# The last 64 keys' high and low parts in one product with V, from block 44 on

## The reference

```
scores = (q @ k.T) / 8
thresh = max(scores, -1) - tau
scores = where(scores >= thresh, scores, -1e9)
attn   = exp(scores - max) ; attn = attn / (sum(attn) + 1e-9)
x      = attn @ v                      -> tokens [2304, 512]
h = x @ w1_in ; x = (h * clip(h + 3, 0, 6) / 6) @ w1_out
h = x @ w2_in ; x = (h * sigmoid(1.702 h))     @ w2_out
```

## Time and profile before

| | us |
|---|---|
| median of the 3 timed runs (1092.23 to 1095.72) | 1092.24 |
| the profiled execution | 1094.09 |
| its span, first to last instruction | 1092.3 |
| PE busy | 1049.8 (96%) |
| DVE busy | 803.6 (74%) |
| ACT busy | 601.6 (55%) |
| POOL busy | 473.4 (43%) |

### The profile page before, as it was taken

One profiled execution on the slowest core, in us unless ns is written; L12 is line 12 of the kernel. 1 busy time (PEld: TensorE's weight loads), 2 busy tenths in 40 slices (PEclk: granted clock), 3 DMA queues, 4 the chain that ended last, 5 costly groups with the idle time before them and its releaser, 6 DMA issues.

```text
span 1092.3 us, 18054 instructions
## 1 busy us (share of the span) xinstructions
PE 1049.8 (96%) x6504; PEld 986.7 (90%) x6504; DVE 803.6 (74%) x1436; ACT 601.6 (55%) x1073; POOL 473.4 (43%) x558
## 2 busy tenths in 40 slices
PE   4888899999999999999999999999999999999998
PEld 3767699999999999899999999998998989898897
DVE  4888978788888878776785747898574798666561
ACT  4888886867777776654451615554251546334240
POOL 3566755455645565435370504146150516324050
PEclk9999999999999999999999999999999999999999
DMA  4446553436335452553225032342303033331302
GB/s 117 126 133 172 146 131 108 111 98 151 91 120 124 133 137 77 128 152 112 83 68 159 16 116 78 101 129 64 110 1 114 22 126 111 101 116 38 108 1 87
DMA packets 102824, 112.41 MB, mean 103 GB/s; under 512 B 28096, under 2 KB 81488, under 8 KB 102736
## 3 DMA queue, kind: packets, MB, share of 16 engines
q1 hardware_dynamic: 102432, 110.97, 35.6%
q10 hardware_dynamic: 304, 0.30, 0.1%
HBM read 78.12 MB, written 33.10 MB: 102 GB/s over the span
## 4 chain that ended last, share of the span: by engine, by line
PE 86%; DVE 6%; issue 3%; ACT 3%; DMA 1%; POOL 1%; SPq 0%; ACTq 0%; DVEq 0%; POOLq 0%
PE score L855 12%; PE score L815 11%; PE mm L815 9%; PE score L736 8%; PE mm L774 7%; PE tr L751 6%; PE tr L855 6%; PE mm L781 6%; PE mm L765 6%; PE score L853 5%; PE tr L815 4%; PE tr L853 2%; PE mm L853 2%; DVE prob L958 2%; PE score L781 2%
## 5 line engine op out<-in xcount | busy, mean ns | idle before, releaser
L1594 POOL TENSOR_TENSOR gd_lo<-act_ring,gd_hi 128x384 fp32r<-128x384 f32 x144 | 157.5, 1114 | 350.1 <-ACT gd_hi L1379 348.3
L1269 ACT ACTIVATE pt_hi<-tr 128x640 fp32r<-128x640 f32 x144 | 101.5, 705 | 99.7 <-PE tr L751 99.2
L950 DVE TENSOR_REDUCE neg_max<-score 128x1 f32<-128x576 f32 x144 | 108.3, 752 | 27.6 <-PE score L736 24.4
L976 DVE TENSOR_TENSOR pt_lo<-tr,pt_hi 128x640 fp32r<-128x640 f32 x144 | 118.2, 821 | 11.2 <-ACT pt_hi L1269 10.4
L736 PE MATMUL score<-k_hi,q_sp 128*128 128x288 f32 x320 | 98.2, 323 | 28.4 <-DVE prob L958 19.5
L1558 POOL TENSOR_SCALAR thresh<-neg_max,tau_abs 128x1 f32<-128x1 f32 x144 | 41.6, 289 | 180.4 <-DVE neg_max L950 179.8
L958 DVE SCALAR_TENSOR_TENSOR prob<-score,thresh,prob 128x576 f32<-128x576 f32 x144 | 116.3, 808 | 0.0
L751 PE MATMUL tr<-ident,prob 128*128 128x128 f32 x720 | 105.8, 279 | 8.5 <-issue 6.8
L1264 ACT ACTIVATE prob<-score,neg_max 128x576 f32<-128x576 f32 x144 | 106.3, 738 | 7.8 <-DVE neg_max L950 7.5
L751 PEld LDWEIGHTS tr<-ident,prob 128*128 128x128 f32 x720 | 83.7, 143 | 19.4 <-issue 18.6
L736 PEld LDWEIGHTS score<-k_hi,q_sp 128*128 128x128 f32 x320 | 62.6, 196 | 39.6 <-DVE prob L958 29.7
(11 more groups left out here) (193 smaller groups left out, 3135.6 us busy)
## 6 DMA issues: line engine op xcount, KB each, us to landing
pair_raw<-x_t_scratch SPq DMA_DIRECT2D x36, 384.0 KB, 3.8
q_raw<-in_qT SPq DMA_DIRECT2D x64, 144.0 KB, 2.8
k_raw<-in_kT SPq DMA_DIRECT2D x62, 144.0 KB, 2.9
raw_a<-in_w_out SPq DMA_DIRECT2D x48, 128.0 KB, 2.2
o_parts_scratch<-o_t SPq DMA_DIRECT2D x32, 160.0 KB, 1.8
x_t_scratch<-x_raw SPq DMA_DIRECT2D x8, 576.0 KB, 3.2
part_t_scratch<-y_out SPq DMA_DIRECT2D x8, 576.0 KB, 3.3
y_ring<-part_t_scratch SPq DMA_DIRECT2D x24, 192.0 KB, 2.7
```

What stands on the lines that cost most here:

```text
L950: dve.tensor_reduce(neg_max[:, r:r + 1], score[:, g % 2, :, 0:HALF], AX.XY, ALU.max, negate=True).then_inc(max_done, 1)
L976: dve.tensor_tensor(pt_place(pt_lo, x), turned_place(x), pt_place(pt_hi, x), ALU.subtract).then_inc(pt_lo_done, 1)
L1269: act.activation(pt_place(pt_hi, x), turned_place(x), ACT.Copy).then_inc(pt_hi_done, 1)
L1594: pool.tensor_tensor(gd_lo[:, u, c, :], act_ring[:, g % 3, :], gd_hi[:, u, c, :], ALU.subtract).then_inc(g_lo_done, 1)
```

## The change

From block 44 on (`stacks`), the tail's two parts share one chunk. POOL copies the last 64 columns of a block's `prob` into the 64 columns behind them (`copy_tail`, new, in POOL's step x + 1 right behind the threshold), so the fifth transpose puts the same 64 keys on partitions 0 to 63 and 64 to 127. PE's turn of such a block waits for that copy. ACT's high part is as before. DVE's low part becomes two instructions: on partitions 64 to 127 of the fifth chunk it writes turned minus high back into `pt_hi`, and on the other four chunks it writes `pt_lo` as before (512 elements per partition, not 640). The fifth chunk of `pt_hi` then holds high parts on top and low parts below; it is multiplied once, in the low part of the group's product: nine matmuls, not ten. V's tail has to stand on both halves too, so `load_v` loads it twice (one DMA more for each head) and the memset of `v_raw` goes.

```
+        def stacks(x):
+            return x >= BATCH_SLOTS + LAG
...
-                sp.dma_start(v_raw[0:TAIL, FULL, :], v[h, full:S, :]).then_inc(v_loaded, 16)
+                for half in range(2):
+                    sp.dma_start(v_raw[half * TAIL:half * TAIL + TAIL, FULL, :], v[h, full:S, :]).then_inc(v_loaded, 16)
...
+                if stacks(x):
+                    pe.wait_ge(tail_copied, x - BATCH_SLOTS - LAG + 1)
...
-                for c in range(CHUNKS):
-                    p_part = (pt_hi, pt_lo)[low]
+                stacked = stacks(group_last(n))
+                for c in range(FULL if stacked and not low else CHUNKS):
+                    p_part = pt_lo if low and not (stacked and c == FULL) else pt_hi
...
-            dve.memset(v_raw[:, FULL, :], 0.0).then_inc(consts_done, 1)
...
+                here, there = slice(0, FULL), slice(FULL, CHUNKS)
+                low = pt_place(pt_hi, x)[TAIL:2 * TAIL, there]
+                dve.tensor_tensor(low, turned_place(x)[TAIL:2 * TAIL, there], low, ALU.subtract)
+                dve.tensor_tensor(pt_place(pt_lo, x)[:, here], turned_place(x)[:, here], pt_place(pt_hi, x)[:, here],
+                                  ALU.subtract).then_inc(pt_lo_done, 1)
...
+            def copy_tail(x):
+                pool.wait_ge(mask_done, x + 1)
+                pool.tensor_copy(prob[:, x % PROBS, S:WIDE], prob[:, x % PROBS, S - TAIL:S]).then_inc(tail_copied, 1)
...
+                if 0 <= g - 1 < G and stacks(g - 1):
+                    copy_tail(g - 1)
```

More of the change, by code:

```diff
@@ L289, in attention_moe_kernel @@
         pt_lo_done = sem("pt_lo_done")
+        tail_copied = sem("tail_copied")
         pv_done = sem("pv_done")
@@ L627, in _ @@
             load_q(1)
-            sp.wait_ge(consts_done, 8)
+            sp.wait_ge(consts_done, 7)
             load_v(0)
@@ L865, in bank_before @@
                 return first_block(d) - 2 + b if d > 0 else None
-            pe.wait_ge(consts_done, 8)
+            pe.wait_ge(consts_done, 7)
             scores(0)
@@ L975, in low_turned @@
                 dve.wait_ge(pt_hi_done, x + 1)
-                dve.tensor_tensor(pt_place(pt_lo, x), turned_place(x), pt_place(pt_hi, x), ALU.subtract
-                                  ).then_inc(pt_lo_done, 1)
+                if not stacks(x):
+                    dve.tensor_tensor(pt_place(pt_lo, x), turned_place(x), pt_place(pt_hi, x), ALU.subtract
+                                      ).then_inc(pt_lo_done, 1)
+                    return
+                here, there = slice(0, FULL), slice(FULL, CHUNKS)
[3 more added lines that the diff above has]
+                                  ALU.subtract).then_inc(pt_lo_done, 1)
             def low_x(ti, k):
@@ L1255, in high_v @@
             def high_v(h):
-                act.wait_ge(v_loaded, 32 * (h + 1))
+                act.wait_ge(v_loaded, 48 * (h + 1))
                 wait(act, pv_done, 4 * (h // 2) if h % 2 else 4 * (h // 2) - 2)
@@ L1403, in _ @@
                 act.dma_start(k_raw[half * HD:half * HD + HD, 0, :], kT[0]).then_inc(k_loaded[0], 16)
-            act.wait_ge(consts_done, 8)
+            act.wait_ge(consts_done, 7)
             act.activation(warm[:, :], three[:, :], ACT.Exp)
@@ L1532, in _ @@
             pool.memset(ident[:, :], 0.0).then_inc(consts_done, 1)
-            pool.wait_ge(consts_done, 5)
+            pool.wait_ge(consts_done, 4)
             pool.affine_select(out=ident[:, :], in_=ident[:, :], compare_op=ALU.not_equal, fill=1.0, base=0,
                                pattern=[[-1, P]], channel_multiplier=1).then_inc(consts_done, 3)
-            pool.wait_ge(consts_done, 8)
+            pool.wait_ge(consts_done, 7)
             pool.wait_ge(tau_done, 6)
```

## The result

| | before | after |
|---|---|---|
| median of the timed runs, taken in turn | 1093.01 us | 1095.47 us |
| lowest to highest | 1091.56 to 1096.44 us | 1093.15 to 1098.73 us |
| profiled execution: time, span | 1094.1 us, 1092.3 us | 1095.70 us, 1093.9 us |

The ratio is 1.0019 with a 95% interval of 1.0012 to 1.0026: about 2.1 us slower. The prediction was 4.0 us faster, with 1092.2 us as its upper end. In the changed kernel's code the lines are: scores L743, turn L760, product with V L775, pieces L784 and L791, row maximum L959, mask L967, the low part L991 (128 elements on partitions 64 to 127, in place) and L992 (512 elements), POOL's copy L1574, threshold L1579.

What follows compares the result with a forecast made beforehand. The prediction took PE to bound the stretch from 137 to 470 us: 4.6 us saved less 0.5 for DVE is 4.1, taken as 4.0, giving 1088.2 us from the median 1092.24; range 1086.0 to 1092.2 us.

Steps and rivals of the forecast that it cites:

- Where it is bound: From 137 to 470 us: a PE-bound stretch with 12 short DVE-bound or ACT-bound places at steps without a piece.
- what is removed: One matmul in each of 45 groups' high halves, at 0.148 or 0.119 us each: 6.0 us.
- where it doesn't count: Eight empty steps where PE waits for the mask lose 1.2 us, two other high halves 0.2: 4.6 us remain.
- DVE's second instruction: Splitting DVE's low part costs 0.07 us a block, 0.15 without overlap; 0.5 us counts on the path.
- the sign that the prediction had named for the rival (0.9): DVE's low part as two instructions takes 0.81 us from start to start; 0.9 would show that DVE takes over.
- The rival that DVE takes over: Saturated stretches at +0.15 a block: 5 x (6 x 0.15 - 0.35) = 2.8 us cost, time 1090.4 us; chance 0.13.
- POOL's copy: POOL's copy of 64 elements takes 0.35 us (0.29 to 0.42), hidden by 0.4 us slack before the turn: 0 us.
- the rival of late copies: POOL copies of 0.86 us make steps 4.3 us against 3.3; about 3 us behind over four, 9 us slower; chance 0.08.
- PE's wait: One more wait on POOL's semaphore for each turn on PE: 0 us, upper bound 2 us.
- SP's third DMA: One more DMA issued by SP for each head, 0.52 us, 16 us over the queue; hidden, 0 us.
- the moved memset: The memset at the start lies beside PE's wait for the first q: 0 us.
- The same length: The stretch from 480 us on stays as long as before and starts 4 us earlier.

Runs made afterwards that it cites:

- e1: Kernel before, with only the matmuls cut from 5 to 4 in each group's high half from block 44 on: ratio 0.9971, 3.2 us less; stretch 316.99 us.
- e2: Kernel before, with DVE's low part split in two instructions from block 44 on, the small one on all 128 partitions: ratio 1.0006, stretch 321.42 us.
- e3: Kernel before, with DVE's low part split in two from block 44 on, the small instruction on partitions 0 to 63: ratio 1.0006, stretch 321.38 us.
- e6: Changed kernel, with DVE's small in-place instruction on all 128 partitions, not 64 to 127: ratio 0.9987 against before, stretch 317.59 us.
- e5: Kernel before, with the low part split in two, the small instruction on partitions 64 to 127, written to pt_lo: ratio 1.005, stretch 324.45 us.
- e4: Kernel before, with only POOL's copy and PE's wait for it from block 44 on: ratio 1.0024, 2.6 us slower; stretch 320.82 us.
- e10: Changed kernel, with two more long-met waits at the start of DVE's queue: ratio 1.0005 against before, stretch 321.11 us.
- e9: Changed kernel, with DVE's small instruction on all 128 partitions as high part times a 0 or -1 factor plus turned: ratio 0.9986 against before, stretch 318.37 us.
- e11: Kernel before plus POOL's copy and PE's wait for it, with 80 more long-met waits on PE before the first scores: ratio 1.0002 against before.

## Why the prediction was wrong, step by step

- **Where it is bound, what is removed, where it doesn't count.** Right. 4.6 us predicted, 4.2 measured by e1 (3.94 in the stretch, 0.30 behind it).
- **DVE's second instruction.** The step that failed. Its price was taken from instructions that start at partition 0, as if the two starts were alike. With that start it holds: e2 and e3 cost 0.5 us, as the sum had it. At partition 64 it costs 0.28 us a block, four times the 0.07, and nearly twice the 0.15 that stood as upper bound. That bound allowed for no overlap with the next instruction but not for a gap ahead of its own start, so it was no bound. From the first instruction's start to the start behind the second it is 0.91 us, the sign that the prediction had named for the rival (0.9); the gap of 0.12 us ahead stood in no sign. On the path, 3.4 us by after against e6 and 3.1 by e5 against e3. The account of the stretch: -3.94 (e1) + 0.60 (e6 against e1: copy and split together) + 3.42 (after against e6) = +0.08 us.
- **The rival that DVE takes over** had the right place and the wrong price. With 0.28 its own formula gives 5 x (6 x 0.28 - 0.35) = 6.7 us of cost and 2.1 slower than before; the runs give 4.0 us (after against e1). A stretch as saturated as that, with 0.3 to 0.4 us of idle time, should have kept its formula open for a price of unknown size, and the range with it.
- **POOL's copy.** Right that it is hidden: no turn waits for it. Its size was below the range, 0.24 us where 0.35 was predicted and 0.29 was the lower end. In the rival of late copies four steps of 4.3 us against 3.3 give 4 us of lateness, not 3; nothing hung on it, as the copy was far shorter than that rival's 0.86 us.
- **PE's wait, SP's third DMA, the moved memset.** PE's wait costs nothing in the stretch (e4: -0.1 us). The DMA and the memset have no run of their own; e6, which has both, is 0.60 us above e1, and e2 alone explains 0.49 of that.
- **Behind the attention.** "The same length" holds from the second dense part to the last matmul, not at either side of it. The 0.59 us ahead of it is DVE's low part again: in the chain the two idle times before turns grow from 0.32 to 0.61 and from 0.96 to 1.14 us, and the last low part with the copy behind it from 1.02 to 1.19, less 0.29 for two shorter high halves; the other 0.2 is a DMA of 2.88 us where before has 2.66.
- **The end of the span.** +1.18 us from an instruction fetch beside the last store. No step of the prediction had it; it alone would have brought the forecast from -4.0 to -2.8. That it stood there in this kernel and not in before is an accident of the instruction count, as far as e10 shows.

Here the chain of the changed kernel at the place of the earlier trace rows, where the high half is shorter and the idle time before the next turn longer:

```profile
459.11 0.74 PE mm L775 x5
459.84 1.14 issue
460.98 0.74 PE tr L760 x5
461.72 0.60 PE mm L775 x4
```

By the rule of the Trainium skill that the prediction weighed (SBUF — State Buffer, "Who interferes with whom"), a VectorE instruction with at most one SBUF input doesn't contend with GpSimd. The trace agrees: L991 and L992 read one operand from PSUM and one from SBUF, and their durations lie within 3 ns of each other in 100 cases each, with POOL at work beside many of them.

## What to carry to other kernels

Price an added instruction by a row with the same partitions as well as the same size, and where there is none, leave the range open by the gap that it may have ahead of itself and behind; it was worth 3.4 us here, of a gain of 3.9. An operation on half of the partitions that starts at 64, between neighbours that start at 0, may cost more than the same on all 128 with a per-partition factor that makes half of it a copy (e9). And with effects of 0.2%, look at how the exposed DMAs lie to the instruction fetches before believing that a change did or didn't pay: two waits took 1.1 us off the end of the profiled execution.

## What the runs showed of the hardware

- A DVE subtract of 128 elements on partitions 64 to 127 started 0.12 us after the instruction ahead of it had begun its accumulator read, and the next one started 0.30 to 0.31 us later (after, e5). Its neighbours start at partition 0 in every run. From partition 0, with 64 or 128 partitions, in place (e6) or not (e2, e3), the two are 0.00 and 0.20 us.
- A POOL copy or cast of 64 elements took 0.24 us, a subtract of 64 elements 0.32 to 0.33; the first copy, in block 44, took 0.24 us like the others.
- An 8 KB instruction fetch beside the last store made it land after 3.2 us instead of 2.0; a 16 KB one beside the store of the last partial outputs, after 2.6 (e1), and with an 8 KB one, after 2.8 and 3.9 (e11, e4), instead of 1.8. Two more waits at the start of DVE's queue moved the 8 KB fetch from 1092.1 to 1083.7 us; 80 more on PE moved the 16 KB one only from 466.7 to 466.1 us.
